# Routing visits of a fused retention, expert and gate kernel moved to the ends of tiles of products

## What is computed

```
logits = x @ w_gate ; order = argsort(-logits.flatten())
for idx in order: token, expert = idx // 8, idx % 8
    if token is free and expert has room: assign
out[mask_e] = relu(x[mask_e] @ w1[e]) @ w2[e]      # 512 -> 1024 -> 512
```

## Time and profile before

| what | us |
|---|---|
| median of the runs | 1139.66 |
| the profiled execution, its own time | 1140.66 |
| its span, first to last instruction | 1138.9 |
| PE busy | 1066.7 (94%) |
| DVE busy | 564.3 (50%) |
| ACT busy | 344.2 (30%) |
| POOL busy | 371.1 (33%) |
| mean granted PE clock | 0.973 of full |

### The profile page before, as it was taken

One profiled execution on the slowest core, in us unless ns is written; L12 is line 12 of the kernel. 1 busy time (PEld: TensorE's weight loads), 2 busy tenths in 40 slices (PEclk: granted clock), 3 DMA queues, 4 the chain that ended last, 5 costly groups with the idle time before them and its releaser, 6 DMA issues.

```text
span 1138.9 us, 20418 instructions
## 1 busy us (share of the span) xinstructions
PE 1066.7 (94%) x7592; PEld 973.4 (85%) x7592; DVE 564.3 (50%) x1431; ACT 344.2 (30%) x659; POOL 371.1 (33%) x363
## 2 busy tenths in 40 slices
PE   5999933989999999999999999999999999999996
PEld 4888812878999989989998899989998999899995
DVE  3555458566355644564456535653556345631111
ACT  2444323322233223322341234123422232224211
POOL 5444301571244123503250325041504151325101
PEclk9999955999999999999999999999999999999998
DMA  9999443311132113212231223121312130304000
GB/s 209 237 243 231 111 120 102 112 38 47 56 103 74 47 56 93 83 39 64 81 96 37 66 66 111 37 66 56 114 31 69 54 113 19 93 23 144 19 1 28
DMA packets 172960, 96.47 MB, mean 85 GB/s; under 512 B 80224, under 2 KB 158048, under 8 KB 172896
## 3 DMA queue, kind: packets, MB, share of 16 engines
q1 hardware_dynamic: 169056, 82.92, 27.6%
q0 software_dynamic: 3840, 12.59, 3.4%
HBM read 82.90 MB, written 12.58 MB: 84 GB/s over the span
## 4 chain that ended last, share of the span: by engine, by line
PE 75%; DVE 8%; issue 2%; POOL 0%; ACT 0%; DMA 0%; DVEq 0%; POOLq 0%
PE bank L1143 19%; PE bank L1145 18%; PE bank L1144 18%; PE bank L1221 6%; PE bank L1222 5%; PE bank L1223 5%; DVE above L879 2%; PE bank L1138 1%; DVE prefix L919 1%; PE bank L1102 1%; PE bank L1110 1%; DVE best L885 0%; DVE top L893 0%; PE bank L1129 0%; ACT ph L811 0%
## 5 line engine op out<-in xcount | busy, mean ns | idle before, releaser
L741 POOL TENSOR_TENSOR ring<-ring_raw,ring 128x512 fp32r<-128x512 f32 x184 | 239.0, 1304 | 432.5 <-ACT ring L791 429.2
L1143 PE MATMUL bank<-h2h,resident 128*128 128x384 f32 x768 | 263.2, 343 | 0.7 <-DVE h2l L1009 0.2
L1145 PE MATMUL bank<-h2h,resident 128*128 128x384 f32 x768 | 258.0, 336 | 0.0
L1144 PE MATMUL bank<-h2l,resident 128*128 128x384 f32 x768 | 257.5, 335 | 0.0
L1143 PEld LDWEIGHTS bank<-h2h,resident 128*128 128x128 f32 x768 | 144.4, 188 | 4.7 <-DVE h2l L1009 1.3
L1144 PEld LDWEIGHTS bank<-h2l,resident 128*128 128x128 f32 x768 | 144.4, 188 | 3.1
L1145 PEld LDWEIGHTS bank<-h2h,resident 128*128 128x128 f32 x768 | 144.1, 188 | 0.0
L791 ACT ACTIVATE ring<-ring_raw 128x512 fp32r<-128x512 f32 x192 | 117.6, 623 | 68.1 <-DMA ring_raw<-in_moe_w_out_dram 43.0
L1018 DVE TENSOR_TENSOR pf<-bank,gate 128x384 f32<-128x384 f32 x96 | 53.1, 554 | 169.4 <-PE bank L1145 165.7
L811 ACT ACTIVATE ph<-pf 128x384 fp32r<-128x384 f32 x96 | 50.4, 525 | 243.0 <-DVE pf L1018 243.0
L807 ACT ACTIVATE gate<-bank 128x384 f32<-128x384 f32 x96 | 47.1, 491 | 214.5 <-PE bank L1145 214.5
(11 more groups left out here) (174 smaller groups left out, 1739.4 us busy)
## 6 DMA issues: line engine op xcount, KB each, us to landing
ring_raw<-in_moe_w_dram SPq DMA_DIRECT2D x128, 256.0 KB, 2.9
ring_raw<-in_moe_w_out_dram SPq DMA_DIRECT2D x64, 256.0 KB, 2.9
qraw<-in_q_dram SPq DMA_DIRECT2D x24, 256.0 KB, 4.4
kraw<-in_k_dram SPq DMA_DIRECT2D x24, 256.0 KB, 4.9
vraw<-in_v_dram SPq DMA_DIRECT2D x24, 256.0 KB, 5.1
xrows<-xrow SPq DMA_DIRECT2D x24, 256.0 KB, 3.2
resident_raw<-in_moe_w_gate_dram SPq DMA_DIRECT2D x12, 256.0 KB, 4.5
resident_raw<-in_moe_w_val_dram SPq DMA_DIRECT2D x12, 256.0 KB, 4.8
```

The costliest lines, as they stand in the source:

```text
L741: nc.gpsimd.tensor_tensor(ring[:, s, 1, :], ring_raw[s][:, :], ring[:, s, 0, :].bitcast(F32), ALU.subtract).then_inc(piece_lo, 1)
L1143: nc.tensor.matmul(ps, wh, xhi, start=start, stop=False)
L1144: nc.tensor.matmul(ps, wh, xlo, start=False, stop=False)
L1145: return nc.tensor.matmul(ps, wl, xhi, start=False, stop=stop)
```

## The change

The five lines that set `visit_at` are replaced. Before, the visits stand at fixed column counts: 6.8 us of columns for a digit, with its visits at 0, 1.7 and 4 us in it. After, the places are taken from the sorted list of tile ends (with the middles of the h2 tiles and the ends of the out products), each at least a set distance behind the one before.

```
-        DIGIT_GAP, LATE_GAP, PART_GAP = us(6.8), us(5), us(4)
-        visit_at = [us(1) + vis // 3 * DIGIT_GAP + us((0, 1.7, 4)[vis % 3]) for vis in range(3 * DIGITS)]
-        visit_at += [visit_at[-1] + (n + 1) * LATE_GAP for n in range(4)]
-        visit_at += [visit_at[-1] + (n + 1) * PART_GAP for n in range(PARTS - 1)]
+        seams = sorted(h_end + h2_half_end + gate_end + val_end + out_end)
+        GAPS = [us(2), us(1.6), us(2)]
+        LATE_GAP, PART_GAP = us(4), us(4)
+        visit_at = []
+        for vis in range(VISITS):
+            gap = GAPS[vis % 3] if vis < V_TIE else LATE_GAP if vis <= V_IDS else PART_GAP
+            wanted = visit_at[-1] + gap if visit_at else 0
+            visit_at.append(min(s for s in seams if s >= wanted))
```

## The result

The changed kernel takes 1158.38 us (median of 4 runs, 1157.56 to 1160.4), the kernel before beside it 1140.53 (4 runs): ratio 1.0158, 95% interval 1.0139 to 1.0178. It is 17.9 us slower. Predicted were 1160, with a range of 1149 to 1173. The rest of this document tests whether the terms of that sum are the true ones. (In the changed kernel the lines behind `visit_at` have moved by 4: L1145 is now L1149, L1221 is L1225, L879 is L883.)

A forecast was written before the change was run, and what follows sets the result against it. PE's own work was taken to bound each round. Rounds 1 to 6 add 10.7, round 0 3.4, the clock 6.4: +20.5 on the median of 1139.66 gives 1160 us, range 1149 to 1173.

The forecast's parts named there:

- Number and place of the visits: nothing: PE's 28 visits, before and after: same matmuls, and standing at a group's end saves nothing.
- the rival: Visits at seams: each saves the slow second product, 0.09 us on all 28, giving 1136 with the clock held; chance 0.04.
- The closing block, +1.61 a round: DVE's work from visit 27, now ahead of product(6): PE waits 2.36 us at out products 6, +1.61 in 7 rounds.
- Visit 9, +0.41 a round: PE at visit 9, one step nearer visit 8: compares delayed by POOL end too late, +0.41 us in each of 7 rounds.
- the bare rule: Shared DVE/POOL port at visit 9: first to start holds it, so the stall would be 0, the sum 2.9 lower.
- Visit 15, -0.24: PE behind visit 15: the wait of gate 0 for the last h2_low goes, -0.24 us a round in rounds 1 to 6.
- Round 0, +3.4 without the clock: Round 0: 0.41 for visit 9, 1.61 for the block and 1.4 for late T0s and out products 0.
- the three late T0: Round 0, POOL busy without a break: three T0s lose up to 0.52 us more each; taken as +1.2.
- The clock, +6.4: PE's clock halves behind one in two of 10 stalls: 5 drops, 1 there before, 1.6 us each; bounds 0 and 14.
- a forecast with the clock held: PE's clock over all rounds: no more drops than now, +14.1, 1154; chance 0.22.
- the one with POOL at every digit: POOL meets the compares at every digit: five more T0s at 0.4 in seven rounds, +14, 1174; chance 0.10.
- the one in which the new stall is hidden: Seams equal other places in cost and the new stall is hidden in some way: 1138 to 1142; chance 0.04.

The follow-up runs named there:

- e1: The changed kernel with visit 27 alone moved one out step later, behind the end of val 6: 1137.22 us, ratio 0.9968 to the kernel before.
- e5: e1 with digit visits 0 to 20 one step (0.52 us) behind their seams: 1161.49 us, ratio 1.0179.
- e11: e5 with DVE's order of e1 restored, its answers to visits 0 to 20 ahead of the same operations as there: 1143.73 us, ratio 1.0021.
- e6: e1 with POOL's piece 14 cut to 64 of its 512 columns, the rest filled with zeros: 1134.79 us, ratio 0.9944.
- e9: e1 with visit 9 alone one step (0.52 us) later, where it stood before: 1134.8 us, ratio 0.9945.
- e8: e1 with POOL's 12 extra low parts of round 0 all moved behind piece 23: 1134.97 us, ratio 0.9946.

## Why the prediction was right, by its steps

*Number and place of the visits: nothing.* Right. Undisturbed T0s take 0.34 us from product to product at a group's end (changed kernel, e1) and inside one (e5, e11), and the second product comes 0.26 us behind the first in all four. So the slow second product, which the rival wanted to save, is there at a seam too.

*The closing block, +1.61 a round.* Right as a mechanism (e1: gone with one visit's place), and the largest. Mis-sized: against round 2, 2.17 - 0.75 = 1.42 and not 1.61. I had taken the whole 9.03 us over; it is 8.83 to 8.85 in the changed kernel. In four rounds of the kernel before (1, 2, 5 and 6) it was 9.02 to 9.04, and there DVE's operation on the digits (L897, now L901) took 0.43 to 0.45 us, beside the last part of POOL's gather; in the other three it took 0.25, as it always does in the changed kernel, where the gather comes behind the block. That the gather is the reason is read from these times and was not tested apart. The operation in round 2 before and in round 1 after:

```profile
525.28 0.45 DVE L897 TENSOR_SCALAR digit_i<-digit_i 128x168 int32<-128x168 int32 x1
...
404.57 0.25 DVE L901 TENSOR_SCALAR digit_i<-digit_i 128x168 int32<-128x168 int32 x1
```

I had noted that the gather would be late, and did not follow it to the block. As the block was not 9.03 in every round before, the seven waits went from 4.8 us in sum to 15.2, by 10.4 where I had 11.3.

*Visit 9, +0.41 a round.* Right: 0.42 in round 1, in six of seven rounds. In round 6 piece 14 landed later, POOL asked when the second compare was running, and nothing was lost. That it is POOL is shown by e6, that the distance matters by e9, and that POOL falls between the compares when visits stand a step off the seams by e11, at three visits of the four named (visit 15 only in some rounds). On the seams, the other T0s of the changed kernel wait for nothing in rounds 1 to 6: POOL comes 1.37 us or more after the product ahead, or is done before the compares, and these end 1.70 to 1.76 after it. I had seen only one form of the meeting. In rounds 0 and 3 POOL's second piece does not follow the first at once but starts 0.94 us after the product ahead instead of 0.46 (in round 3 ACT waited 1.1 us for its data). `prefix` gets through, and the second compare waits instead, here in round 3, for the same 0.41:

```profile
581.06 0.25 DVE L923 SCALAR_TENSOR_TENSOR prefix<-prefix,bank,digit_f 128x24 f32<-128x24 f32 x1 [1.23 <-PE bank L1118]
581.35 2.13 DVE L883 TENSOR_TENSOR above<-prefix,ladder 128x384 bf16<-128x384 f32 x2
...
581.61 1.45 POOL L745 TENSOR_TENSOR ring<-ring_raw,ring 128x512 fp32r<-128x512 f32 x1 [0.48 <-ACT ring L795]
```

The Trainium skill's rule on the shared port (SBUF — State Buffer, Who interferes with whom) was tested here. That the loser waits for the whole instruction agrees: in round 1 `prefix` ends 0.03 us after POOL's two operations (340.02 + 2.54 = 342.56), in round 3 the second compare 0.42 after POOL's one, about its own length. That a GpSimd instruction which only writes is no obstacle for two SBUF inputs agrees too: in e6 the compares took 1.03 us beside the fill. What the prediction held against the bare rule stands: where two of POOL's operations were back to back (seven rounds of the kernel before, four of the changed one), the waiting `prefix` never got in between and took 1.35 us.

*Visit 15, -0.24.* Right: T0's cost there fell to 0.17 in each of rounds 1 to 6. It had been 0.14 to 0.27 above that, 1.4 us in sum, as I had it.

*Round 0, +3.4 without the clock.* The block gave 1.6, visit 9 0.4, the three late T0 only 0.3 together; about 2.3. What I took for them (0.52 less distance, so 1.2 more) counts only if all else stands still, and POOL's long run of work meets them at other moments.

*The clock, +6.4.* Right in sum, five falls against one, each worth 119.9 - 118.3 = 1.6. It rested on one case in three and was a guess at "one in two" of ten stalls. It came out as five of seven at `pl` and none of three among the digits of round 0. That it fits in sum is luck; a forecast with the clock held, which I gave 0.22, would have been 6 us lower.

The sum was 20.5: the block was 0.9 too high over seven rounds, visit 9 0.4 (round 6), round 0 1.1. That leaves 18.1, and the rounds of the two profiled executions differ by 961.9 - 943.6 = 18.3 us (17.9 is the difference of the medians). Of the rivals, the one with the clock holding (1154) is out by the PEclk column, the one with POOL at every digit by the timelines, the one of faster visits at seams by the 0.34 and 0.26 us of the products behind them, and the one in which the new stall is hidden by the seven waits of 2.17.

## What to carry to other kernels

Where work is put into an engine's fixed order by comparing it with due times, look at what stands behind it at equality: one visit that ties with the end of a tile put 6.5 us of DVE work ahead of the operation that PE needed next. Ending a side chain earlier is worth nothing when nothing waits for it, and its last and longest block belongs right behind a due piece, not ahead of one. For such a change read three things in each period: when the other engines' requests arrive, which of two engines that hold each other up asks first, and how long the main engine is left without work, as a wait of 2 us can cost another 1.6 in clock.

## What was not expected of the hardware

- The clock: waits for `pl` that lost 2.17 us, between products without a gap, were followed by 3.4 us at half clock in 5 of 7 cases in each of two kernels; waits for `pl` that lost 1.64 us in none of 7. Why two of seven escaped, and why two stalls of 2.48 us in round 0 did too, was not tried.
- A wait moved from one chain of DVE to another gives back little: 12 POOL operations held up three T0s by 6.1 us in sum (e1), or one chain of ties by 4.4 (e8).
- Moving the 21 digit visits by 0.52 us moved the time by 24 us (e1 to e5), of which the order of DVE's queue was 17.8 (e5 to e11) and the rest, mostly the meeting with POOL, 6.5 (e11 to e1).
